# Top-32 attention and two MLPs: inverse row sums once per group, through HBM

## The chip, the cores and the metric

The kernel runs on one core of a Trainium2 chip. The metric is the device time of one execution in microseconds; three executions of the kernel before took 1342.15, 1345.45 and 1345.49 us, median 1345.45. Five engines take part: PE (TensorE: matmuls and transposes), DVE (VectorE), ACT (ScalarE), POOL (GpSimd) and SP (SyncE), which issues every DMA of this kernel. Each runs its own queue of instructions in the order written and waits for others by semaphores.

## The reference

```python
scores = scale * np.matmul(q, k.transpose(0, 1, 3, 2))        # (4, 8, 576, 576), head_dim 64
kth = np.partition(scores, -32, axis=-1)[..., -32:-31]
scores = np.where(scores >= kth, scores, -1e9)
scores = scores - np.max(scores, axis=-1, keepdims=True)
attn = np.exp(scores)
attn = attn / (np.sum(attn, axis=-1, keepdims=True) + 1e-09)
x = np.matmul(attn, v)            # heads side by side: (2304, 512)
y = (sigmoid(x @ w_gate) * (x @ w_val)) @ w_out               # d_ff 1536
out = np.maximum(y @ w_in, 0) ** 2 @ w_out2                   # d_ff 2048
```

All is float32. Only row sums of the exponentials concern us here: each query row of each head has one, and row q of x must be multiplied by its inverse.

## The kernel before

**Tiling.** The 2304 tokens are cut into five chunks of 320, 512, 512, 512 and 448 columns. x is kept with its 512 features on partitions (four head pairs, two heads of 64 features each) and tokens along the free dimension. A *group* (32 of them) is one head pair of one batch within a chunk, 2 to 7 blocks of 64 queries. A group is cut into *units* (80): 128 queries of both heads, or, where the number of blocks is odd, a last half unit of 64 queries. A full unit has two *tiles* (one per head, 128 queries on the partitions), a half unit one (64 queries of head 0 on partitions 0 to 63, of head 1 on 64 to 127). There are 144 tiles. `END[u]` is the last tile of unit u, `FINAL_UNIT[g]` the last unit of group g.

**Slots.** All engines run the same loop over 148 slots; slot s belongs to tile s, whose score matmul PE issues two slots ahead. DVE finds the 32 largest in slots s and s+1 (four MAX8, three MATCH_REPLACE). In slot s+2 ACT (`find_below`, `enlarge`), POOL (`mask`) and ACT (`exp`, which also gives the row sums, L528) make the exponentials. In slot END+3 PE transposes the unit (`turn`, nine transposes, L404), ACT copies the result to SBUF (`copy_pt`) and PE multiplies by v (`times_v`, L422 and L424).

**Normalisation before.** Exponentials put queries on partitions, x puts them along the free dimension, so the inverse must be turned as well. Per unit, in slot END+3: POOL adds 1e-9 (`add_eps`, L719), DVE inverts (`invert`, L649), POOL spreads the two inverses over 128 columns (`spread_inverse`, L729), PE transposes that (L412), in `times_v`, ahead of the products with v. It lands in the same PSUM bank, RR, as the product. In slot END+4 ACT copies both, 256 columns, to `rp` (`copy_pv`, L543), and POOL multiplies them into `xf` (`normalise`, L738; for a half unit two multiplies of 64x64, L743 and L746). When a pair has all its columns in a chunk, ACT and POOL split xf into a high and a low part (`split_x`, L555 and L752, at the slot in `X_AT`), the inputs of the three-pass products.

**MLP.** A chunk's products (68 weight blocks, each in two halves of six matmuls, L465 to L467) run beside the attention of the next chunk. `shares()` deals the 136 halves to the slots so that PE's work per slot is even by a cost formula written in the program; a slot's share has three parts (before the scores, before times_v, after it). Products of chunk c begin in slot `MLP_AT[c]` (23, 56, 88, 120, 147); the last chunk's, `REST`, run after the last slot. A block's results are evacuated by ACT, DVE and POOL, for the third part in the next slot. Weights are split into high and low parts once: for chunks 0 and 1 some blocks are split on the way (ACT L549, POOL L707) and stored to HBM (L322); otherwise both parts are loaded (L329) into a ring of four places, each when the block four before is done.

**Order on the engines around the change.** POOL in a slot: add_eps, normalise, mask, split_x, evac of the last third part, spread_inverse, split_head, split_weights, evac. ACT: copy_scores, find_below, copy_pv, enlarge, evac of the last third part, copy_pt, split_x, exp, split_head, split_weights, evac. SP: ring loads and stores of the last third part, loads of heads and v, raw weights and their stores, ring loads of parts one and two.

## Time and profile before

| | us |
|---|---|
| median of three executions | 1345.45 |
| profiled execution, its own time | 1344.6 |
| its span, first to last instruction | 1342.8 |
| DVE busy | 846.0 (63%) |
| ACT busy | 808.0 (60%) |
| POOL busy | 731.5 (54%) |

TensorE's mean granted clock was 0.94 of full speed. An engine's busy share says how full it is on average, and averages hide stages: the first stretch holds attention alone, the last one matmuls alone. Times "from 380 us" and the like count from the start of the span. A row of a group view reads: line, engine, operation, what it writes and reads, shape, count, then busy us and mean ns of one, then the idle time of the engine just ahead of them with what ended most of it.

### The profile page before, as it was taken

The page shows a single profiled execution, that of the slowest core. Times are in us where ns is not written, and L with a number is a line of the kernel's source. Part 1 is how long each engine was busy: PE and PEld are TensorE (multiplying, and loading weights), DVE is VectorE, ACT ScalarE, POOL GpSimd, SP SyncE. Part 2 cuts the span into 40 slices and gives each one's busy share as a digit, 9 for nine tenths or more (in the row PEclk, how much of TensorE's full clock was granted, in tenths as well). Part 3 has the DMA queues.
Part 4 walks back from the last instruction along what each step waited for, and adds up shares of the span by engine and source line. Part 5 has one row for each costly group of instructions (what it writes and reads, how often), then busy time and mean ns, then how long its engine had stood idle before and what let it go on. Part 6 is the DMA issues. An engine that isn't in the chain of part 4 may idle for free.

```text
span 1342.8 us, 20893 instructions
## 1 busy us (share of the span) xinstructions
PE 1205.0 (90%) x6960; PEld 1033.2 (77%) x6960; DVE 846.0 (63%) x1680; ACT 808.0 (60%) x1712; POOL 731.5 (54%) x785
## 2 busy tenths in 40 slices
PE   3465588887789999999999999999999999999999
PEld 3344487877687888877888888788888887889998
DVE  6767877777876775787757868875666676011130
ACT  5667777667776676777656657755565574311130
POOL 5766577777775664787536527854453553122130
PEclk9655789898899999999999999999999999999999
DMA  4666145555465556545655555656454544566665
GB/s 135 224 234 216 58 159 208 178 176 177 159 221 211 210 186 214 194 171 197 214 181 178 183 165 194 211 165 219 149 195 160 184 139 151 160 219 216 216 216 184
DMA packets 78873, 249.34 MB, mean 186 GB/s; under 512 B 8752, under 2 KB 9776, under 8 KB 78768
## 3 DMA queue, kind: packets, MB, share of 16 engines
q1 hardware_dynamic: 78768, 248.02, 54.3%
q8 instruction: 56, 0.92, 0.3%
q14 instruction: 49, 0.40, 0.1%
HBM read 207.62 MB, written 40.37 MB: 185 GB/s over the span
## 4 chain that ended last, share of the span: by engine, by line
PE 69%; POOL 16%; ACT 7%; issue 6%; DMA 2%; SPq 0%; POOLq 0%; ACTq 0%
PE ps L465 18%; PE ps L467 18%; PE ps L466 17%; PE ps L422 5%; PE ps L404 4%; PE ps L392 4%; POOL ring L707 4%; POOL below L712 4%; POOL klo L694 3%; POOL qkh L699 2%; PE ps L424 2%; ACT qkh L500 2%; POOL full_buf L773 1%; DMA w_raw<-w_in 1%; ACT scores L505 1%
## 5 line engine op out<-in xcount | busy, mean ns | idle before, releaser
L465 PE MATMUL ps<-xy_hi,ring 128*128 128x512 f32 (+2 forms) x800 | 306.1, 383 | 15.2 <-POOL ring L707 7.3
L633 DVE MAX8 top<-work 128x8 f32<-128x576 f32 x432 | 312.4, 751 | 5.0
L466 PE MATMUL ps<-xy_lo,ring 128*128 128x512 f32 (+2 forms) x800 | 297.5, 372 | 0.0
L467 PE MATMUL ps<-xy_hi,ring 128*128 128x512 f32 (+2 forms) x800 | 297.5, 372 | 0.0
L712 POOL TENSOR_TENSOR below<-scores,below 128x576 f32<-128x576 f32 x144 | 206.9, 1437 | 58.3 <-ACT below L517 51.1
L465 PE MATMUL ps<-g_hi,ring 128*128 128x512 f32 (+2 forms) x560 | 214.2, 382 | 7.7 <-POOL ring L707 7.5
L635 DVE MATCH_REPLACE8 work<-top,work 128x576 f32<-128x576 f32 x288 | 214.0, 743 | 0.0
L467 PE MATMUL ps<-g_hi,ring 128*128 128x512 f32 (+2 forms) x560 | 208.8, 373 | 0.0
L466 PE MATMUL ps<-g_lo,ring 128*128 128x512 f32 (+2 forms) x560 | 208.6, 373 | 0.0
L465 PEld LDWEIGHTS ps<-xy_hi,ring 128*128 128x128 f32 x800 | 152.6, 191 | 35.8 <-issue 8.6
L467 PEld LDWEIGHTS ps<-xy_hi,ring 128*128 128x128 f32 x800 | 151.8, 190 | 22.4
L466 PEld LDWEIGHTS ps<-xy_lo,ring 128*128 128x128 f32 x800 | 152.5, 191 | 17.3
L528 ACT ACTIVATE probs<-below,nbias 128x576 f32<-128x576 f32 x128 | 100.3, 784 | 103.0 <-POOL below L712 102.7
L694 POOL TENSOR_TENSOR klo<-raw,qkh 128x576 fp32r<-128x576 f32 x64 | 91.4, 1428 | 110.0 <-ACT qkh L500 109.8
L659 DVE SCALAR_TENSOR_TENSOR full_buf<-act_buf,ps 128x512 f32<-128x512 f32 (+2 forms) x60 | 37.9, 632 | 169.9 <-PE ps L467 163.2
L707 POOL TENSOR_TENSOR ring<-w_raw,ring 128x512 fp32r<-128x512 f32 x90 | 116.6, 1300 | 38.0 <-ACT ring L549 36.0
L763 POOL TENSOR_TENSOR g_lo<-full_buf,g_hi 128x512 fp32r<-128x512 f32 (+2 forms) x60 | 70.9, 1182 | 106.4 <-ACT g_hi L583 105.8
L670 DVE TENSOR_TENSOR g_lo<-full_buf,g_hi 128x512 fp32r<-128x512 f32 (+2 forms) x80 | 75.1, 939 | 82.6 <-ACT g_hi L587 82.6
L392 PE MATMUL ps<-qkh 128*128 128x288 f32 x320 | 101.2, 330 | 28.1 <-ACT scores L505 17.4
L773 POOL TENSOR_TENSOR full_buf<-act_buf 128x512 f32<-128x512 f32 (+2 forms) x80 | 83.2, 1042 | 76.4 <-ACT act_buf L576 74.4
L465 PEld LDWEIGHTS ps<-g_hi,ring 128*128 128x128 f32 x560 | 107.0, 191 | 21.6 <-POOL ring L707 4.6
L467 PEld LDWEIGHTS ps<-g_hi,ring 128*128 128x128 f32 x560 | 106.5, 190 | 15.8
(56 smaller groups left out, 2118.8 us busy)
## 6 DMA issues: line engine op xcount, KB each, us to landing
ring<-w_split SPq DMA_DIRECT2D x273, 512.0 KB, 3.4
w_split<-ring SPq DMA_DIRECT2D x68, 512.0 KB, 2.9
w_raw<-w_in SPq DMA_DIRECT2D x90, 256.0 KB, 3.5
vt<-v_in SPq DMA_DIRECT2D x32, 320.0 KB, 4.8
raw<-qk_in SPq DMA_DIRECT2D x16, 512.0 KB, 4.9
raw<-qk_in SPq DMA_DIRECT2D x16, 416.0 KB, 4.5
raw<-qk_in SPq DMA_DIRECT2D x8, 576.0 KB, 4.5
raw<-qk_in SPq DMA_DIRECT2D x8, 480.0 KB, 4.7
```

Of the source, the lines that this page charges most:

```text
L392: mm = nc.tensor.matmul(dst, qkh[:, r, at:at + P], rhs, start=(done == 0), stop=(done == steps - 1))
L465: nc.tensor.matmul(dst, w_hi, hi[:, k, 0:WIDTH[c]], start=(k == 0), stop=False)
L466: nc.tensor.matmul(dst, w_hi, lo[:, k, 0:WIDTH[c]], start=False, stop=False)
L467: mm = nc.tensor.matmul(dst, w_lo, hi[:, k, 0:WIDTH[c]], start=False, stop=(k == parts * KT - 1))
L528: last = nc.scalar.activation(probs_of(u)[rows, h, :], below[rows, t % 2, :], ACT.Exp, bias=nbias[rows, t % 4:t % 4 + 1], scale=SCALE, acc ...
L633: nc.vector.max(out=best, in_=sc if step == 0 else wk).then_inc(sel_step[t % 2], 1)
L635: nc.vector.match_replace(out=wk, in_to_replace=best, in_values=sc if step == 1 else wk, imm_value=-3.0e38).then_inc(sel_step[t % 2], 1)
L670: nc.vector.tensor_tensor(out=g_lo[:, j, 0:n_w], in0=full_buf[:, j % 2, 0:n_w], in1=g_hi[:, j, 0:n_w].bitcast(F32), op=ALU.subtract).then_ ...
L694: nc.gpsimd.tensor_tensor(out=klo[:, j % 4, :], in0=raw[:, j % 2, q:q + SEQ], in1=qkh[:, j % 4, q:q + SEQ].bitcast(F32), op=ALU.subtract). ...
L707: nc.gpsimd.tensor_tensor(out=place(k)[:, 1, :], in0=w_raw[:, r % RAW, :], in1=place(k)[:, 0, :].bitcast(F32), op=ALU.subtract).then_inc(w ...
L712: nc.gpsimd.tensor_tensor(out=below[:, t % 2, :], in0=scores[:, t % 4, :], in1=below[:, t % 2, :], op=ALU.subtract).then_inc(mask_done, 1)
L773: nc.gpsimd.tensor_tensor(out=full_buf[:, j % 2, 0:n_w], in0=act_buf[:, j % 2, 0:n_w], in1=act_buf[:, j % 2, 0:n_w], op=ALU.mult).then_inc ...
```

## The change

Per unit, PE no longer transposes inverses, and `copy_pv` copies 128 columns of the unnormalised product from PSUM straight into xf (for a half unit, two copies of 64x64). The row sums of a group are collected in 2 to 7 columns of `rsum`. Once per group: POOL adds 1e-9 and DVE inverts, at the end of its slot END+3 of the group's last unit; SP stores the inverses in slot END+4 to a table `inv` in HBM (queries along the row), and at the end of the same slot loads them back with two or four DMAs, each repeated over the 64 partitions of its head, into `rr`; POOL multiplies the group's columns of xf by `rr` in place, in slot END+5 (for group 3, the last of chunk 0, in slot END+4, which is slot 23).

The order of the engines' work moves too. POOL masks first, and evacuates before it normalises. ACT's copy_pv comes after enlarge and after evac of the last third part. X_AT follows the groups' normalisation: chunk 0's pairs are split in slots 9, 14, 19 and 23 (before: 8, 13, 18, 23), the last pairs of chunks 1, 2 and 3 in slots 56, 88 and 120 (before: 55, 87, 119). The last chunk's products start a slot later, so that the number of slots is 149. In slot 23 the whole share of products is put after times_v.

```diff
@@ -115,8 +125,8 @@
 
 
 
-MASK, TURN, NORM = 2, 3, 4
-MLP_AT = [CHUNK_END[c] + (4 if c in (0, NC - 1) else 5) for c in range(NC)]
+MASK, TURN, COPY = 2, 3, 4
+MLP_AT = [CHUNK_END[c] + (4 if c == 0 else 5) for c in range(NC)]
 SLOTS = MLP_AT[NC - 1] + 1
...
@@ -141,8 +151,7 @@
             upto = min(max(upto, done), 2 * NB)
             todo = [(c, h) for h in range(done, upto)]
             done = upto
-            a = (len(todo) + 1) // 3
-            b = (len(todo) + 1) // 3
+            a = b = 0 if s == MLP_AT[0] else (len(todo) + 1) // 3
             out[s] = (todo[:a], todo[a:a + b], todo[a + b:])
...
-HEADS_AT, X_AT = {}, {}
+HEADS_AT, NORM_AT, X_AT = {}, {}, {}
 for _g in range(1, NG):
     for _h in range(2):
         HEADS_AT.setdefault(max(FIRST_TILE[_g] - 4 + _h, 0), []).append((_g, _h))
+for _g in range(NG):
+    NORM_AT.setdefault(END[FINAL_UNIT[_g]] + (4 if _g == PAIRS - 1 else 5), []).append(_g)
 for _c in range(NC):
     for _p in range(PAIRS):
-        _s = END[X_UNIT[_c][_p]] + NORM
+        _s = next(s for s in NORM_AT if X_GROUP[_c][_p] in NORM_AT[s])
         X_AT.setdefault(_s if _c == 0 else max(_s, slot_of_block(_c - 1, OUT0 - 1) + 1), []).append((_c, _p))
...
+INV_AT = {END[FINAL_UNIT[g]]: g for g in range(NG)}
...
-        rsum = sb("rsum", [P, 2, 2])
-        rsum_eps = sb("rsum_eps", [P, 2, 2])
-        rinv = sb("rinv", [P, 2, 2])
-        rinv_q = sb("rinv_q", [P, 2, 2, B64])
+        rsum = sb("rsum", [P, 2, NBLK])
+        rsum_eps = sb("rsum_eps", [P, 2, NBLK])
+        rinv = sb("rinv", [P, 2, NBLK])
+        rr = sb("rr", [P, 2, NMAX])
         pt = sb("pt", [P, 2, NBLK * P])
-        rp = sb("rp", [P, 2, 2 * P])
...
+            def store_inverses(g):
+                n = sums_of(g)
+                sp.wait_ge(inv_done, g + 1)
+                sp.dma_start(inv[g, 0:n, :].rearrange("m q -> q m"), rinv[:, g % 2, 0:n],
+                             allow_slow_non_contiguous=True).then_inc(inv_stored, 16)
+
+            def load_inverses(g):
+
+                n = GROUPS[g][4] // 2
+                sp.wait_ge(inv_stored, 16 * (g + 1))
+                wait(sp, x_done, g - 1)
+                for h in range(2):
+                    rows = slice(DH * h, DH * h + DH)
+                    if n:
+                        sp.dma_start(rr[rows, g % 2, 0:P * n].rearrange("p (i q) -> p i q", q=P),
+                                     inv[g, h:2 * n:2, :].unsqueeze(0).to_broadcast([DH, n, P])).then_inc(
+                                         inv_loaded[g % 2], 16)
+                    if GROUPS[g][4] % 2:
+                        sp.dma_start(rr[rows, g % 2, P * n:P * n + B64],
+                                     inv[g, 2 * n:2 * n + 1, B64 * h:B64 * h + B64].to_broadcast([DH, B64])).then_inc(
+                                         inv_loaded[g % 2], 16)
...
             for s in range(SLOTS):
                 if s > 0:
                     mlp_dma(blocks_of(SHARES[s - 1][2]))
+                if s - COPY in INV_AT:
+                    store_inverses(INV_AT[s - COPY])
...
                 mlp_dma(blocks_of(SHARES[s][0] + SHARES[s][1]))
+                if s - COPY in INV_AT:
+                    load_inverses(INV_AT[s - COPY])
...
                 for k in range(NBLK):
-                    dst = ps[:, T0 + k // 4, P * (k % 4):P * (k % 4) + P] if k < 8 else ps[:, RR, 0:P]
-                    mm = nc.tensor.transpose(dst, both[:, P * k:P * k + P], ident[:, :])
+                    mm = nc.tensor.transpose(ps[:, T0 + k // 4, P * (k % 4):P * (k % 4) + P], both[:, P * k:P * k + P], ident[:, :])
                 mm.then_inc(transposed, 1)
 
             def times_v(u):
                 g = UNITS[u][1]
                 pe.wait_ge(pt_copied, u + 1)
-
-                pe.wait_ge(inv_spread, u + 1)
-                nc.tensor.transpose(ps[:, RR, 0:P], rinv_q[:, u % 2, :, :].rearrange("p h c -> p (h c)"),
-                                    ident[:, :]).then_inc(inv_turned, 1)
...
                 wait(act, transposed, u - 1)
-                wait(act, sum_done, u - 1)
+                wait(act, sum_done, g - 1)
...
                     rows = slice(B64 * h, B64 * h + B64) if part == 2 else slice(0, P)
-                    col = 0 if part == 2 else h
+                    col = 2 * i if part == 2 else 2 * i + h
                     last = nc.scalar.activation(probs_of(u)[rows, h, :], below[rows, t % 2, :], ACT.Exp,
                                                 bias=nbias[rows, t % 4:t % 4 + 1], scale=SCALE,
-                                                accum_out=rsum[rows, u % 2, col:col + 1])
...
             def copy_pv(u):
+                c, g, p, i, half, col = UNITS[u]
                 act.wait_ge(pv_done, u + 1)
-                wait(act, x_done, u - 1)
-                nc.scalar.activation(rp[:, u % 2, :], ps[:, RR, 0:PV + P], ACT.Copy).then_inc(pv_copied, 1)
+                if c > 0:
+
+                    act.wait_ge(x_lo_done, (c - 1) * NM + p + 1)
+                for h in range(2) if half else [2]:
+                    rows = slice(DH * h, DH * h + DH) if half else slice(0, P)
+                    at, n = (PV + B64 * h, B64) if half else (PV, P)
+                    last = nc.scalar.activation(xf[rows, p, col:col + n], ps[rows, TAIL, at:at + n], ACT.Copy)
+                last.then_inc(pv_copied, 1)
...
@@ -597,12 +638,12 @@
                     copy_scores(s + 1)
                 if 0 <= s - MASK < NT:
                     find_below(s - MASK)
-                if s - NORM in UNIT_AT:
-                    copy_pv(UNIT_AT[s - NORM])
                 if 0 <= s - MASK < NT:
                     enlarge(s - MASK)
                 for c, n in blocks_of(SHARES[s - 1][2]) if s else []:
                     evac(c, n)
+                if s - COPY in UNIT_AT:
+                    copy_pv(UNIT_AT[s - COPY])
                 if s - TURN in UNIT_AT:
                     copy_pt(UNIT_AT[s - TURN])
...
-            def invert(u):
-                heads = 1 if UNITS[u][4] else 2
-                dve.wait_ge(sum_done, u + 1)
-                wait(dve, inv_spread, u - 1)
-                nc.vector.reciprocal(rinv[:, u % 2, 0:heads], rsum_eps[:, u % 2, 0:heads]).then_inc(inv_done, 1)
+            def invert(g):
+                n = sums_of(g)
+                dve.wait_ge(sum_done, g + 1)
+                if g >= 2:
+                    dve.wait_ge(inv_stored, 16 * (g - 1))
+                nc.vector.reciprocal(rinv[:, g % 2, 0:n], rsum_eps[:, g % 2, 0:n]).then_inc(inv_done, 1)
...
@@ -676,12 +718,12 @@
                 select_both(s, [0, 1])
                 for c, n in blocks_of(SHARES[s - 1][2]) if s else []:
                     evac(c, n)
-                if s - TURN in UNIT_AT:
-                    invert(UNIT_AT[s - TURN])
                 select_both(s, [2])
                 for c, n in blocks_of(SHARES[s][0] + SHARES[s][1]):
                     evac(c, n)
                 select_both(s, [3])
+                if s - TURN in INV_AT:
+                    invert(INV_AT[s - TURN])
...
-            def add_eps(u):
-                heads = 1 if UNITS[u][4] else 2
-                pool.wait_ge(exp_done, END[u] + 1)
-                wait(pool, inv_done, u - 1)
-                nc.gpsimd.tensor_scalar(rsum_eps[:, u % 2, 0:heads], rsum[:, u % 2, 0:heads], 1e-9, None,
+            def add_eps(g):
+                n = sums_of(g)
+                pool.wait_ge(exp_done, END[FINAL_UNIT[g]] + 1)
+                wait(pool, inv_done, g - 1)
+                nc.gpsimd.tensor_scalar(rsum_eps[:, g % 2, 0:n], rsum[:, g % 2, 0:n], 1e-9, None,
                                         ALU.add).then_inc(sum_done, 1)
 
-            def spread_inverse(u):
-                pool.wait_ge(inv_done, u + 1)
-                wait(pool, inv_turned, u - 1)
-                if UNITS[u][4]:
-                    src = rinv[:, u % 2, 0:1].unsqueeze(2).to_broadcast([P, 2, B64])
-                else:
-                    src = rinv[:, u % 2, :].unsqueeze(2).to_broadcast([P, 2, B64])
-                nc.gpsimd.tensor_copy(rinv_q[:, u % 2, :, :], src).then_inc(inv_spread, 1)
-
-            def normalise(u):
-                c, g, p, i, half, col = UNITS[u]
-                pool.wait_ge(pv_copied, u + 1)
...
-                    pool.wait_ge(x_lo_done, (c - 1) * NM + p + 1)
-                if not half:
-                    nc.gpsimd.tensor_tensor(out=xf[:, p, col:col + P], in0=rp[:, u % 2, PV:PV + P],
-                                            in1=rp[:, u % 2, 0:P], op=ALU.mult).then_inc(x_done, 1)
...
-
-                pool.wait_ge(inv_spread, u + 1)
-                nc.gpsimd.tensor_tensor(out=xf[0:B64, p, col:col + B64], in0=rp[0:B64, u % 2, PV:PV + B64],
-                                        in1=rp[0:B64, u % 2, 0:B64], op=ALU.mult).then_inc(x_half_done, 1)
-                pool.wait_ge(x_half_done, RANK[u] + 1)
-                nc.gpsimd.tensor_tensor(out=xf[B64:P, p, col:col + B64], in0=rp[B64:P, u % 2, PV + B64:PV + P],
-                                        in1=rp[B64:P, u % 2, B64:P], op=ALU.mult).then_inc(x_done, 1)
-                pool.wait_ge(x_done, u + 1)
+            def normalise(g):
+                c, b, p, at, n, col = GROUPS[g]
+                pool.wait_ge(pv_copied, FINAL_UNIT[g] + 1)
+                pool.wait_ge(inv_loaded[g % 2], 16 * inv_loads(g))
+                x = xf[:, p, col:col + B64 * n]
+                nc.gpsimd.tensor_tensor(out=x, in0=x, in1=rr[:, g % 2, 0:B64 * n], op=ALU.mult).then_inc(x_done, 1)
...
             for s in range(SLOTS):
-                if s - TURN in UNIT_AT:
-                    add_eps(UNIT_AT[s - TURN])
-                if s - NORM in UNIT_AT:
-                    normalise(UNIT_AT[s - NORM])
                 if 0 <= s - MASK < NT:
                     mask(s - MASK)
+                if s - TURN in INV_AT:
+                    add_eps(INV_AT[s - TURN])
+                for c, n in blocks_of(SHARES[s - 1][2]) if s else []:
+                    evac(c, n)
+                for g in NORM_AT.get(s, []):
+                    normalise(g)
                 for c, p in X_AT.get(s, []):
                     split_x(c, p)
-                for c, n in blocks_of(SHARES[s - 1][2]) if s else []:
-                    evac(c, n)
-                if s - TURN in UNIT_AT:
-                    spread_inverse(UNIT_AT[s - TURN])
                 for g, h in HEADS_AT.get(s, []):
                     split_head(g, h)
...
```

## Rows read from the trace of the kernel before

**Rows 1.** The page, part 1: busy us (share of the span) xinstructions by engine.

```profile
PE 1205.0 (90%) x6960; PEld 1033.2 (77%) x6960; DVE 846.0 (63%) x1680; ACT 808.0 (60%) x1712; POOL 731.5 (54%) x785
```

**Rows 2.** Windows: length, busy PE, PEld, DVE, ACT, POOL, then PEclk, DMA share, GB/s.

```profile
0.00:170.00 170.00, 90.79 (x475) 73.68 (x476) 119.38 (x246) 113.68 (x237) 107.81 (x123) 0.68 0.50 171
170.00:380.00 210.00, 170.84 (x1195) 159.81 (x1194) 163.87 (x330) 151.76 (x340) 158.38 (x167) 0.91 0.52 181
380.00:1190.00 810.00, 793.55 (x4556) 661.22 (x4555) 539.08 (x1076) 512.30 (x1079) 438.82 (x470) 0.99 0.54 186
1190.00:1343.00 153.00, 149.82 (x740) 138.52 (x738) 23.62 (x29) 30.28 (x59) 26.46 (x26) 1.00 0.64 209
```

**Rows 3.** The chain of waits from 0 to 200 us, by line.

```profile
by line: issue 15.2%; POOL below L712 11.9%; POOL ring L707 11.9%; DMA w_raw<-w_in 7.9%; POOL klo L694 7.1%; POOL qkh L699 6.0%; ACT qkh L500 5.7%; PE ps L404 3.8%; ACT scores L505 3.0%; ACT below L510 2.7%; DMA raw<-qk_in 1.9%; PE ps L392 
```

**Rows 4.** PE's waits from 170 to 380 us: us in total, times, longest us.

```profile
PE ps L412 <- POOL rinv_q L729: 23.3, 9, 5.7
PE ps L465 <- POOL ring L707: 12.2, 6, 4.8
```

**Rows 5.** PE's waits from 380 to 1190 us.

```profile
PE ps L412 <- POOL rinv_q L729: 9.8, 5, 2.8
PE ps L465 <- DMA ring<-w_split: 1.1, 1, 1.1
```

**Rows 6.** Timeline of PE, two places: start us, us, engine, line, operation.

```profile
769.24 1.14 PE L404 MATMUL ps<-ident,probs 128*128 128x128 f32 x9
770.13 0.48 PE L465 MATMUL ps<-g_hi,ring 128*128 128x512 f32 x1
...
773.31 0.39 PE L467 MATMUL ps<-g_hi,ring 128*128 128x512 f32 x1
773.54 0.27 PE L412 MATMUL ps<-ident,rinv_q 128*128 128x128 f32 x1
773.74 1.09 PE L422 MATMUL ps<-pt,vt 128*64 128x128 f32 x16
```

**Rows 7.** Groups of POOL instructions, 170 to 380 us: busy us, mean ns, idle before.

```profile
L738 POOL TENSOR_TENSOR xf<-rp 128x128 f32<-128x128 f32 x14 | 6.7, 480 | 13.3 <-ACT rp L543 13.2
L729 POOL COPY rinv_q<-rinv 128x128 f32<-128x128 f32 x14 | 4.3, 309 | 0.1
L719 POOL TENSOR_SCALAR rsum_eps<-rsum 128x2 f32<-128x2 f32 x14 | 3.0, 213 | 1.2
```

**Rows 8.** Groups by form over the whole span.

```profile
L712 POOL TENSOR_TENSOR below<-scores,below 128x576 f32<-128x576 f32 x144 | 206.9, 1437 | 58.3 <-ACT below L517 51.1
L752 POOL TENSOR_TENSOR xy_lo<-xf,xy_hi 128x512 fp32r<-128x512 f32 x12 | 15.7, 1313 | 0.9 <-ACT xy_hi L555 0.9
L569 ACT ACTIVATE act_buf<-ps 128x512 f32<-128x512 f32 x36 | 21.4, 593 | 39.6 <-PE ps L467 39.6
L743 POOL TENSOR_TENSOR xf<-rp 64x64 f32<-64x64 f32 x16 | 5.5, 343 | 21.0 <-ACT rp L543 20.9
L752 POOL TENSOR_TENSOR xy_lo<-xf,xy_hi 128x320 fp32r<-128x320 f32 x4 | 3.5, 862 | 0.0
```

**Rows 9.** Timeline around slot 23.

```profile
164.43 0.39 ACT L543 ACTIVATE rp<-ps 128x256 f32<-128x256 f32 x1 [0.64 <-PE ps L424]
...
167.95 0.41 PE L465 MATMUL ps<-xy_hi,ring 128*128 128x320 f32 x1 [2.25 <-POOL xy_lo L752]
```

**Rows 10.** The page, parts 3 and 6: DMA queue, and issues with us to landing.

```profile
q1 hardware_dynamic: 78768, 248.02, 54.3%
...
ring<-w_split SPq DMA_DIRECT2D x273, 512.0 KB, 3.4
w_split<-ring SPq DMA_DIRECT2D x68, 512.0 KB, 2.9
```

**Rows 11.** SP's waits over the span.

```profile
SPq L322 <- POOL ring L707: 395.3, 67, 17.9
```

**Rows 12.** Timeline of SP's issues near 614 us.

```profile
614.46 0.33 SPq L318 DMA_DIRECT2D w_raw<-w_in  x1
```

More of the change, by code:

```diff
@@ L56, with sums_of, inv_loads @@
 RANK = [sum(UNITS[v][4] == UNITS[u][4] for v in range(u)) for u in range(NU)]
-X_UNIT = [[max(u for u in range(NU) if UNITS[u][0] == c and UNITS[u][2] == p) for p in range(PAIRS)] for c in range(NC)]
+X_GROUP = [[max(g for g in range(NG) if GROUPS[g][0] == c and GROUPS[g][2] == p) for p in range(PAIRS)] for c in range(NC)]
 CHUNK_END = [max(END[u] for u in range(NU) if UNITS[u][0] == c) for c in range(NC)]
+def sums_of(g):
+    return 2 * (GROUPS[g][4] // 2) + GROUPS[g][4] % 2
+def inv_loads(g):
+    return sum(2 * ((GROUPS[h][4] > 1) + GROUPS[h][4] % 2) for h in range(g % 2, g + 1, 2))
 def full_columns(g):
@@ L178, with attention_mlps @@
     SPLIT_AT.setdefault(3 + _i // 2, []).append(_k)
-def attention_mlps(nc, qk, v, w, w_split, out):
+INV_AT = {END[FINAL_UNIT[g]]: g for g in range(NG)}
+def attention_mlps(nc, qk, v, w, w_split, inv, out):
     with ExitStack() as ctx:
@@ L217, in attention_mlps @@
         ps = ctx.enter_context(nc.psum_tensor("ps", [P, 8, 512], F32))
-        T0, RR, PV, ACC0 = 2, 4, P, 5
+        T0, TAIL, PV, ACC0 = 2, 4, P, 5
         def s_ps():
@@ L264, in attention_mlps @@
         inv_done = sem("inv_done")
-        inv_spread = sem("inv_spread")
-        inv_turned = sem("inv_turned")
+        inv_stored = sem("inv_stored")
+        inv_loaded = [sem("inv_loaded0"), sem("inv_loaded1")]
         transposed = sem("transposed")
@@ L270, in attention_mlps @@
         pv_copied = sem("pv_copied")
-        x_half_done = sem("x_half_done")
         x_done = sem("x_done")
@@ L421, in times_v @@
                         p_at = P * ((KFULL + 1) * h + k)
-                        nc.tensor.matmul(ps[d, RR, PV:PV + P], vt[:, g % 2, v_at:v_at + DH],
+                        nc.tensor.matmul(ps[d, TAIL, PV:PV + P], vt[:, g % 2, v_at:v_at + DH],
                                          pt[:, u % 2, p_at:p_at + P], start=(k == 0), stop=False)
-                mm = nc.tensor.matmul(ps[:, RR, PV:PV + P], vt[:, g % 2, KFULL * DH:KFULL * DH + P],
+                mm = nc.tensor.matmul(ps[:, TAIL, PV:PV + P], vt[:, g % 2, KFULL * DH:KFULL * DH + P],
                                       pt[:, u % 2, P * KFULL:P * KFULL + P], start=False, stop=True)
@@ L537, in copy_pt @@
                 nc.scalar.activation(pt[:, u % 2, 512:1024], ps[:, T0 + 1, :], ACT.Copy)
-                nc.scalar.activation(pt[:, u % 2, 1024:NBLK * P], ps[:, RR, 0:P], ACT.Copy).then_inc(pt_copied, 1)
+                nc.scalar.activation(pt[:, u % 2, 1024:NBLK * P], ps[:, TAIL, 0:P], ACT.Copy).then_inc(pt_copied, 1)
             def copy_pv(u):
+                c, g, p, i, half, col = UNITS[u]
                 act.wait_ge(pv_done, u + 1)
-                wait(act, x_done, u - 1)
-                nc.scalar.activation(rp[:, u % 2, :], ps[:, RR, 0:PV + P], ACT.Copy).then_inc(pv_copied, 1)
+                if c > 0:
[5 more added lines that the diff above has]
+                last.then_inc(pv_copied, 1)
             def split_weights(k):
@@ L551, in split_x @@
             def split_x(c, p):
-                act.wait_ge(x_done, X_UNIT[c][p] + 1)
+                act.wait_ge(x_done, X_GROUP[c][p] + 1)
                 if c > 0:
@@ L589, in _ @@
             act.wait_ge(const_ready, 1)
-            nc.scalar.activation(rp[:, 0, 0:1], ident[:, 0:1], ACT.Exp)
+            nc.scalar.activation(rsum[:, 0, 0:1], ident[:, 0:1], ACT.Exp)
             split_head(0, 0)
@@ L847 @@
     w_split = nc.dram_tensor("w_split", (NB, P, 2 * KT * P), F32, kind="Internal").ap()
-    attention_mlps(nc, *aps, w_split, out)
+    inv = nc.dram_tensor("inv", (NG, NBLK, P), F32, kind="Internal").ap()
+    attention_mlps(nc, *aps, w_split, inv, out)
     r = run_bass_kernel_spmd(nc, [arrays], core_ids=[0])
```

4 lines of the change are left out of this document (2 added, 2 removed).

## The prediction, made before the result was known

> **What bounds the kernel now.** I read the page's busy times first: PE is busy 1205.0 of 1342.8 us [rows 1]. Then busy time by stretch [rows 2]: there are two regimes. From 380 us to the end of attention (1190) PE is busy 793.6 of 810 us, and after that only matmuls remain; there, what PE issues is what the kernel takes. Before 380 no engine is full. From 0 to 170 us (attention alone, slots 0 to 22) PE has 90.8, DVE 119.4, ACT 113.7, POOL 107.8; from 170 to 380 (chunk 0's products beside chunk 1's attention) PE has 170.8 of 210, DVE 163.9, POOL 158.4. The chain of waits for the first 200 us [rows 3] is led by POOL's mask and weight splits, by "issue" (hand-offs), and by DMA. So POOL's queue, in its order, sets the early pace. PE's own waits say the same: from 170 to 380 it stood 23.3 us at L412, the transpose of the spread inverse, for POOL's rinv_q, and 12.2 us for a weight split [rows 4]; after 380 only 9.8 us at L412 [rows 5].
>
> **The change, part by part.**
>
> *PE, after 380 us.* L412 goes, once per unit; 26 of its 80 executions start before 380 us (14 from 170 on, [rows 7], 12 before that), 54 after. In the gapless stream its start and the next matmul's are 773.54 and 773.74, so one is worth 0.20 us [rows 6]: 54 x 0.20 = 10.8 us off. The stalls in front of it (9.8 us) go too, but the matmuls behind may find a later cause; from 0 to 9.8 I take 6. Together -16.8.
>
> *POOL, 170 to 380.* Fourteen units lose add_eps (3.0 us), spread (4.3) and normalise (6.7), and normalise's 13.3 us of waiting for ACT's copy [rows 7]: 27.3. Seven groups of 256 columns gain an add_eps (0.21) and one normalise. No multiply of 128x256 is in the trace; it lies between 0.48 (128 columns, [rows 7]) and 0.86 (a subtraction of 320, [rows 8]); I take 0.74, near the upper. That is 6.7. POOL's queue gets 20.6 us shorter, but DVE's 163.9 and PE's 170.8 of 210 are close behind and ACT's hand-offs stay. Bounds 0 and 20.6; I take -12.
>
> *POOL, 0 to 170.* Twelve units, four of them half units with two 64x64 multiplies (0.34 each, [rows 8]): 12 x 0.52 + 8 x 0.48 + 4 x 0.68 = 12.8 off; on: 4 x (0.21 + 0.86) = 4.3. Net 8.5, of which the weight loads and ACT's chain hide part: bounds 0 and 8.5, taken -6. Here the mask also comes ahead of anything that waits for PE's product.
>
> *DVE and ACT.* The reciprocals fall from 80 to 32. DVE is no bound (846 of 1342.8 us busy), so I count nothing. ACT's copy shrinks from 256 to 128 columns (0.39 us before, [rows 9]), hidden beside PE after 380 and inside the halves taken above before it.
>
> *The round trip, where it is in the open.* Group 3 ends in slot 19, its inverse is ready at the end of DVE's slot 22, and slot 23 holds store, loads, normalise, split_x and the first matmul. Before, the copy was released at 164.4 and PE began chunk 0 at 167.95, after normalise, high and low split [rows 9]. Now a store must land before the loads are issued. No DMA so small is in the trace; big ones land in 2.9 us (store) and 3.4 (ring load) [rows 10]. Store and load are then 6.3, less the mask that runs beside (1.4, [rows 8]): +5, bounds 0 and 9. It stands in POOL's and ACT's queues: behind it are the splits of the next heads and exp of tile 21, and PE waits for both. In a sentence of its own: the Trainium skill ("DMA: Bandwidth & Descriptors", section "Anatomy of one DMA") gives every DMA about 2 us, mostly the receipt of the write, so by it the round trip would be 4 us and this term 2.6; the two landings in [rows 10] include moving 512 KB, so trace and rule do not contradict each other.
>
> *Other loads in POOL's way.* SP issues load_inverses at the end of its slot, after store_parts, and store_parts waits for POOL's weight split (395 us of SP waiting, [rows 11]). So in slots 8 and 13 and in chunk 0's product slots the loads start only when POOL ends that slot; POOL's next one holds a mask (1.4) and perhaps one block before normalise, against two issues of 0.33 us each [rows 12] and some 3.4 of landing. I take 2 us at slots 9 and 14 and 0.5 for each of eight groups: +8, bounds 0 and 20.
>
> *A new order on ACT.* copy_pv moves behind enlarge and behind the evacuation of the last slot's third share. In slots where a half unit follows at once, PE's turn waits for that very copy at the slot's start (its products share bank TAIL). After 380 there are 12 such slots; in 9 the third share ends in a block on which ACT has no work or in no block. In the other 3 (gate 8, h 14, h 8) ACT must evacuate (0.59, [rows 8]), make a high part of like length and copy (about 0.3), with hand-offs 1.7 us: +5, bounds 0 and 12.
>
> *Starts of chunks 1 to 3.* normalise and split_x of the last pair now stand in the very slot (56, 88, 120) in which PE starts the chunk. PE gets to the second half block, which needs the pair, after nine transposes (769.24 to 770.13), six matmuls of 0.23 [rows 6] and a score: 2.8 us. ACT takes the transposes' copies (about 1.5 us) first, then the high split (near the evacuation's 0.59), then POOL 1.31 [rows 8]: 0.9 + 1.5 + 0.6 + 1.3 + 0.2 = 4.5. Stall 1.7 each, 5 in all. The last chunk's start moves a slot back: loads after the second share, 4 + 1.1 + 0.6 + 1.1 = 6.8 us (multiply, high split and low split of 448 columns, from the rows of 320 and 512), against 4.1 of third share and 1.8 of matmuls that don't need this pair: +1. Bounds 0 and 12 together.
>
> *SP and the DMA queues.* The store writes sums that lie 4 bytes in a partition to addresses 512 bytes apart: 128 x (2 to 7) pieces, none next to another. Over 32 groups that is 18,432 pieces, and the loads are 10,240 of 256 or 512 bytes, on top of 78,768. Price of a 4-byte packet: the trace has none alone; below it costs nothing, above it costs as much as the mean one, 54.3% x 16 x 1342.8 / 78,768 = 0.148 us [rows 10]. A store with 5 sums is 40 packets in each of 16 queues: 0 to 5.9 us ahead of a ring load. A ring load has three blocks to land, 3 x 12 x 0.23 = 8.3 us, less its 3.4: 4.9 in hand. I take a third of the upper price, so 2 us (2.8 for 7 sums): hidden after 380, +2 in all before it. Again by itself: the Trainium skill (same page, "Specifications") says transfers under 512 bytes are a read-modify-write and lose line rate; no row here shows one. If that brought the price to the upper bound, it is the second rival below.
>
> **The sum**: -16.8 - 12 - 6 + 5 + 8 + 5 + 6 + 2 = -8.8. The profiled execution took 1344.6 us (span 1342.8 and 1.8 around it), 0.85 under the median 1345.45. So 1336.6; I say 1336.
>
> **Rivals.**
> 1. *POOL was the whole early bound.* Then its relief counts fully (-20.6 - 8.5), all L412 stalls go (-9.8), and the loads arrive in time (+2 in place of 8, +4 in place of 11): -10.8 - 9.8 - 29.1 + 5 + 2 + 4 + 2 = -37, about 1308. For: 23.3 us of PE waits for POOL at one line. Against: DVE at 164 of 210.
> 2. *The store's packets delay the ring loads (slower).* At 0.148 us the stores of groups 12 to 15 (5.9 us), 20 to 23 (7.1) and 28 to 31 (8.3) exceed the 4.9 in hand by 1.0, 2.2 and 3.4 us, four times each: 26, and some 8 for raw weight loads before 380. 1336 + 34 = 1370. It decides from 4.9 / 56 = 0.09 us per packet. For: a DMA share of 0.54 after 380 [rows 2] with queues shared by all loads. Against: the payload is nearly nothing.
> 3. *POOL's relief is worth nothing* (ACT's chain and DVE hold the early pace) and the round trips stay: -16.8 + 26 = +9, 1355. For: 'issue' and DMA in [rows 3]. Against: [rows 4].
> 4. *Gains and costs cancel*: half of the relief taken, everything added as summed: 1345.
>
> **Chances.** Forecast 0.45, rival 1 0.17, rival 4 0.17, rival 2 0.10, rival 3 0.11. What a measurement can tell from no change is 0.3%, or 4 us. Faster by more than that 0.62, within 0.17, slower 0.21. The range 1314 to 1357 leaves out most of rivals 1 and 2.
>
> **What would show it.** PE from 380 on: no L412, stream gapless before L422, and its length about 11 us less; stalls at L404 for ACT's copy in three slots, at L465 for xy_lo in slots 56, 88, 120. In slot 23 PE's start of chunk 0 relative to the last product's end: 3.5 us before, some 8.5 after. POOL's normalise waiting for DMA in slots 9 and 14. The attention-only stretch shorter by a few us, 170 to 380 by 5 to 12. The landing time of the store (over 5 us speaks for rival 2) and PE's waits for ring loads (1.1 us after 380, [rows 5]) would overturn it, as would an early stretch of unchanged length.

## The result: 1506 us, 12% slower, and the profile after

The changed kernel takes 1506.11 us (median of four executions, 1500.35 to 1507.95), the kernel before 1345.24: a ratio of 1.119, 95% interval 1.116 to 1.123. The prediction said 1336 and 1357 at most.

Windows of the changed kernel, to be read beside [rows 2] (length, busy PE, PEld, DVE, ACT, POOL, PEclk, DMA share, GB/s; its span is 1504.6 us):

```profile
0.00:170.00 170.00, 75.96 (x378) 62.20 (x378) 107.92 (x217) 97.77 (x204) 90.17 (x80) 0.63 0.60 170
170.00:380.00 210.00, 143.89 (x969) 133.86 (x969) 125.54 (x258) 125.13 (x281) 116.82 (x108) 0.83 0.58 134
380.00:1190.00 810.00, 709.01 (x4013) 588.35 (x4014) 514.40 (x1002) 480.16 (x1030) 398.61 (x338) 0.94 0.63 172
1190.00:1505.00 315.00, 300.35 (x1521) 260.79 (x1519) 94.33 (x159) 102.11 (x215) 78.73 (x69) 0.98 0.62 182
```

Before, PE was busy 90.8, 170.8 and 793.6 us in the first three windows; now 76.0, 143.9 and 709.0. No engine took over the work: PE, DVE, ACT and POOL are all less busy in each of the three. Only the DMA share rose (0.54 to 0.63 after 380 us) while the GB/s fell (186 to 172). PE's waits over the span (us in total, times, longest):

```profile
PE ps L430 <- ACT scores L538: 63.4, 20, 10.8
PE ps L498 <- DMA ring<-w_split: 49.0, 19, 9.6
PE ps L498 <- POOL xy_lo L773: 34.8, 5, 14.0
PE ps L441 <- ACT xf L583: 33.1, 13, 5.1
```

They have no single cause: PE stands for scores, for ring loads, for x's low part and for the copied product. Gone, as forecast, is its longest wait of the kernel before:

```profile
PE ps L412 <- POOL rinv_q L729: 49.1, 24, 5.7
```

Now who holds the other engines. POOL's wait ahead of normalise, and SP's ahead of the loads:

```profile
POOL xf L769 <- DMA rr<-inv: 259.2, 31, 27.8
```

```profile
SPq L373 <- DMA inv<-rinv: 141.7, 28, 8.6
```

POOL stood 259 us for the returned inverses, in 31 of 32 groups, and SP 142 us for the stores to land. The chain of work that ended last, by line (the page's part 4), says it too:

```profile
DMA inv<-rinv 14%; PE ps L498 11%; PE ps L499 11%; PE ps L500 11%; DMA rr<-inv 7%; DMA ring<-w_split 6%; POOL ring L749 3%; POOL klo L736 3%; PE ps L441 3%; POOL below L754 3%; POOL qkh L741 2%; PE ps L430 2%; PE ps L455 2%; ACT qkh L533 2%; DMA w_raw<-w_in 1%
```

Here "DMA inv<-rinv" is the store. One round trip in the timeline, group 3 in slot 23 (start us, us, engine, line, operation), against [rows 9]:

```profile
182.26 0.19 DVE L691 RECIPROCAL rinv<-rsum_eps 128x5 f32<-128x5 f32 x1 [5.64 <-POOL rsum_eps L761]
182.47 0.38 SPq L362 DMA_DIRECT2D inv<-rinv  x1
182.89 0.52 SPq L319 DMA_DIRECT2D raw<-qk_in  x1
...
193.91 0.61 SPq L373 DMA_DIRECT2D rr<-inv  x1
...
198.96 0.86 POOL L769 TENSOR_TENSOR xf<-xf,rr 128x320 f32<-128x320 f32 x1 [10.97 <-DMA rr<-inv]
199.85 0.47 ACT L596 ACTIVATE xy_hi<-xf 128x320 fp32r<-128x320 f32 x1 [13.03 <-POOL xf L769]
200.40 0.86 POOL L773 TENSOR_TENSOR xy_lo<-xf,xy_hi 128x320 fp32r<-128x320 f32 x1 [0.58 <-ACT xy_hi L596]
201.31 0.64 PE L498 MATMUL ps<-xy_hi,ring 128*128 128x320 f32 x1 [13.99 <-POOL xy_lo L773]
```

The store is issued at 182.47 and SP can issue the first load at 193.91, 11.4 us later; the inverses are in at 199. PE, through nine of the twelve matmuls of its first block, stood 14.0 us where it stood 2.25 before. POOL stood 11.0 us and ACT 13.0, and behind them are the masks and exponentials of the tiles in work. In all 32 groups the first load is issued 8.8 to 12.8 us after the store. SP has other work in between, so this bounds the landing from above, but 28 times the store is what SP stood for last.

The stall has a second price. The same 320-column matmul before and behind it:

```profile
186.00 0.31 PE L499 MATMUL ps<-xy_lo,ring 128*128 128x320 f32 x1
...
201.75 0.47 PE L499 MATMUL ps<-xy_lo,ring 128*128 128x320 f32 x1
```

From 201.3 to 205 us the granted clock is 0.57 of full speed, near the lower of its two levels (1.2 and 2.4 GHz); from 205 to 210 it is 1.00 again. What that adds up to is counted below, at no_round_trip. DMA of the page, against [rows 10]:

```profile
q1 hardware_dynamic: 109488, 252.82, 61.4%
...
ring<-w_split SPq DMA_DIRECT2D x273, 512.0 KB, 3.8
...
vt<-v_in SPq DMA_DIRECT2D x32, 320.0 KB, 11.0
```

The v loads, which SP issues right behind a store, land in 11.0 us in the median (4.8 before).

### The profile page after: what moved, and what is told of

Same layout as the page of the kernel before. It is cut to its first block, busy times and chain, and to the rows that moved or that the text cites. A ratio compares the mean times of both kernels' runs of the same rounds, so it can differ in the third digit from the quotient of the medians.

```text
span 1504.6 us, 20395 instructions
## 1 busy us (share of the span) xinstructions
PE 1229.2 (82%) x6880; PEld 1045.2 (69%) x6880; DVE 842.2 (56%) x1632; ACT 805.2 (54%) x1728; POOL 684.3 (45%) x593
## 4 chain that ended last, share of the span: by engine, by line
PE 40%; DMA 28%; POOL 13%; ACT 8%; SPq 5%; issue 5%; DVE 0%; ACTq 0%; POOLq 0%
DMA inv<-rinv 14%; PE ps L498 11%; PE ps L499 11%; PE ps L500 11%; DMA rr<-inv 7%; DMA ring<-w_split 6%; POOL ring L749 3%; POOL klo L736 3%; PE ps L441 3%; POOL below L754 3%; POOL qkh L741 2%; PE ps L430 2%; PE ps L455 2%; ACT qkh L533 2%; DMA w_raw<-w_in 1%
## 5 line engine op out<-in xcount | busy, mean ns | idle before, releaser
L498 PE MATMUL ps<-xy_hi,ring 128*128 128x512 f32 (+2 forms) x800 | 313.9, 392 | 99.9 <-DMA ring<-w_split 35.7
L499 PE MATMUL ps<-xy_lo,ring 128*128 128x512 f32 (+2 forms) x800 | 303.9, 380 | 0.0
L500 PE MATMUL ps<-xy_hi,ring 128*128 128x512 f32 (+2 forms) x800 | 303.1, 379 | 0.0
L498 PEld LDWEIGHTS ps<-xy_hi,ring 128*128 128x128 f32 x800 | 156.6, 196 | 127.1 <-issue 56.0
L498 PE MATMUL ps<-g_hi,ring 128*128 128x512 f32 (+2 forms) x560 | 217.3, 388 | 25.9 <-DMA ring<-w_split 13.3
L500 PE MATMUL ps<-g_hi,ring 128*128 128x512 f32 (+2 forms) x560 | 210.9, 377 | 0.0
L500 PEld LDWEIGHTS ps<-xy_hi,ring 128*128 128x128 f32 x800 | 156.3, 195 | 23.2
L499 PEld LDWEIGHTS ps<-xy_lo,ring 128*128 128x128 f32 x800 | 157.1, 196 | 17.9
L430 PE MATMUL ps<-qkh 128*128 128x288 f32 x320 | 105.5, 342 | 73.3 <-ACT scores L538 63.4
L769 POOL TENSOR_TENSOR xf<-xf,rr 128x320 f32<-128x320 f32 (+5 forms) x32 | 25.6, 801 | 259.3 <-DMA rr<-inv 259.2
L674 DVE MAX8 top<-scores 128x8 f32<-128x576 f32 x144 | 107.3, 745 | 61.6 <-ACT scores L538 61.6
L498 PEld LDWEIGHTS ps<-g_hi,ring 128*128 128x128 f32 x560 | 109.4, 195 | 42.1 <-issue 14.4
L712 DVE TENSOR_TENSOR g_lo<-full_buf,g_hi 128x512 fp32r<-128x512 f32 (+2 forms) x80 | 75.8, 948 | 109.7 <-ACT g_hi L628 109.6
L430 PEld LDWEIGHTS ps<-qkh 128*128 128x128 f32 x320 | 70.3, 220 | 83.6 <-issue 72.6
```

The source lines that it names most:

```text
L430: mm = nc.tensor.matmul(dst, qkh[:, r, at:at + P], rhs, start=(done == 0), stop=(done == steps - 1))
L498: nc.tensor.matmul(dst, w_hi, hi[:, k, 0:WIDTH[c]], start=(k == 0), stop=False)
L499: nc.tensor.matmul(dst, w_hi, lo[:, k, 0:WIDTH[c]], start=False, stop=False)
L500: mm = nc.tensor.matmul(dst, w_lo, hi[:, k, 0:WIDTH[c]], start=False, stop=(k == parts * KT - 1))
L674: nc.vector.max(out=best, in_=sc if step == 0 else wk).then_inc(sel_step[t % 2], 1)
L712: nc.vector.tensor_tensor(out=g_lo[:, j, 0:n_w], in0=full_buf[:, j % 2, 0:n_w], in1=g_hi[:, j, 0:n_w].bitcast(F32), op=ALU.subtract).then_ ...
```

## Experiments

The theories about the time lost: **A**, the round trip comes late into queues that work in order; **B**, the store's 4-byte packets hold up all other transfers; **C**, the new order on ACT and POOL and the later starts of the chunks cost the time; **D**, the loads are late by themselves. Each run's time is a median; the kernel before took 1345.0 to 1345.6 beside them.

**no_round_trip**: the whole change but its DMAs and the waits on them; x is multiplied by a constant, so the result is not the reference's.

```diff
-                    store_inverses(INV_AT[s - COPY])
-                    load_inverses(INV_AT[s - COPY])
-                pool.wait_ge(inv_loaded[g % 2], 16 * inv_loads(g))
+            nc.gpsimd.memset(rr[:, :, :], 1.0)
```

> The changed kernel without the store, the loads and the waits on them; x is multiplied by a constant tile instead of the inverses. What is left is the gain side and the new order of work. Theory A (the round trip of the inverses is late, and POOL and SP stand in order behind it) and theory B (the store's 4-byte packets hold up all other transfers) both expect the sum of my prediction without its DMA terms: 1320 us, from 1305 to 1335. Theory C (the new order on POOL and ACT and the later starts of the chunks cost the time) expects over 1450.

Measured: 1324.5 us, ratio 0.985 (0.983 to 0.988): 20.5 us faster than before, where A and B expected it. C falls. Its windows, and PE's waits between 380 and 1175 us:

```profile
0.00:170.00 170.00, 89.55 (x459) 74.02 (x460) 122.27 (x246) 114.28 (x242) 101.38 (x91) 0.73 0.50 171
170.00:380.00 210.00, 179.28 (x1246) 168.61 (x1246) 167.19 (x333) 157.25 (x354) 156.38 (x142) 0.91 0.55 191
380.00:1190.00 810.00, 792.05 (x4526) 658.93 (x4525) 530.73 (x1028) 506.58 (x1084) 406.53 (x339) 1.00 0.54 188
```

```profile
PE ps L437 <- ACT xf L579: 9.9, 8, 2.3
PE ps L494 <- POOL xy_lo L766: 1.3, 2, 0.7
PE ps L494 <- DMA ring<-w_split: 0.2, 1, 0.2
```

From 170 to 380 PE does 8.4 us more work than before in the same stretch, and of the stalls I had charged, little more than the one for ACT's copy is there (9.9 us). Over the whole span, though, other waits of PE have grown:

```profile
PE ps L426 <- ACT scores L534: 30.9, 18, 3.2
PE ps L437 <- ACT xf L579: 23.0, 12, 3.9
PE ps L451 <- ACT pt L568: 15.7, 16, 2.2
```

In the kernel before, the waits for these three were 17.4, 6.2 and 0.4 us. So 45.6 us came back of the 49.1 that went with L412.

This run also tells how the 182 us between it and the changed kernel divide, as PE has the same instructions in both. Part 1 of the page (busy us, share of the span, instructions), in the changed kernel and then here:

```profile
PE 1229.2 (82%) x6880; PEld 1045.2 (69%) x6880; DVE 842.2 (56%) x1632; ACT 805.2 (54%) x1728; POOL 684.3 (45%) x593
```

```profile
PE 1193.5 (90%) x6880; PEld 1024.1 (77%) x6880; DVE 842.0 (64%) x1632; ACT 804.4 (61%) x1728; POOL 687.3 (52%) x594
```

Of the 179 us between the two profiled spans PE stood 143 longer, and for 36 it was busy longer with the same work, at a mean granted clock of 0.90 against 0.95.

**store_only**: the stores without the loads.

```diff
 (against no_round_trip)
+                    store_inverses(INV_AT[s - COPY])
+                    dve.wait_ge(inv_stored[g % 2], 16 * (g // 2))
```

> As no_round_trip, but the 32 stores of the inverses are issued where they were; nobody waits for them but DVE, two groups later. No loads; x is multiplied by a constant tile. Theory A: within 10 us of no_round_trip. Theory B: most of the 185 us between 1320 and 1506 comes back, over 1430.

Measured: 1393.8 us. Neither expectation: 69 us over no_round_trip, so B is real and less than half of the 182 us to explain. The DMA queue and the v loads, first in no_round_trip, then here:

```profile
q1 hardware_dynamic: 78768, 248.02, 53.7%
...
vt<-v_in SPq DMA_DIRECT2D x32, 320.0 KB, 4.7
```

```profile
q1 hardware_dynamic: 97712, 248.10, 62.8%
...
vt<-v_in SPq DMA_DIRECT2D x32, 320.0 KB, 11.1
```

18,944 packets more (18,432 pieces, and 16 for each of the 32 stores) took (62.8% x 1389.7 - 53.7% x 1325.6) x 16 = 2,570 us of the engines, 0.136 us each for 4 bytes. The same sum differs by some 200 us between the kernel before and order_only (below; 54.3% and 53.4%), whose DMAs are the same, so the price is good to about 0.01 us.

**store_only_act_queue**: store_only with the same stores issued by ACT, behind copy_pt.

```diff
 (against store_only)
-                sp.dma_start(inv[g, 0:n, :].rearrange("m q -> q m"), ...
+                act.dma_start(inv[g, 0:n, :].rearrange("m q -> q m"), ...
```

> store_only (1394, v loads landing in 11.1 us against 4.7 without the store), with the same 4-byte stores issued from ACT's DMA queue instead of SP's, at the same slot after copy_pt. If the transfers behind a store are late because they stand behind it in the same queue, they pass it now: v loads near 5 us and 1325 to 1345. If the packets occupy the 16 DMA engines whichever queue they come from: the loads stay late and the time over 1375.

Measured: 1421.6 us. Another queue doesn't help, it costs 28 us more. PE was busy 21.5 us longer than in store_only (1218.6 against 1197.1), at a mean granted clock of 0.92 against 0.94; what brought that about no run settles. The two queues:

```profile
q1 hardware_dynamic: 78768, 248.02, 61.7%
q10 hardware_dynamic: 18944, 0.08, 0.8%
```

This is the clearest row on B. The 18,944 small packets of q10 are recorded with 0.8% of the time, 10 ns each; but q1's 78,768 packets, the same as in no_round_trip, take 61.7% x 1422.5 in place of 53.7% x 1325.6: 2,650 us of the engines more. So the price of the small writes is recorded in the others' packets.

**loads_only**: the loads without the stores, reading w in place of inv. What comes back are not the inverses.

```diff
-                sp.wait_ge(inv_stored, 16 * (g + 1))
-                                     inv[g, h:2 * n:2, :].unsqueeze(0)...
+                                     w[g, h:2 * n:2, 0:P].unsqueeze(0)...
```

> The changed kernel without the stores; the same 96 loads in the same places, waited for by POOL as before, but reading the weights' tensor, so that SP waits for no store. The values in rr are not the inverses. Theory A, with the store's 11 us in the trace as the price: POOL's wait for the loads falls from 259 us to under 60, and the time to 1320 to 1350. Theory B: the same, since the packets of the store are gone. Theory D (the loads themselves, issued at the end of SP's slot, are the late part): over 1400.

Measured: 1360.4 us, 36 over no_round_trip; POOL still stood 87 us:

```profile
POOL xf L764 <- DMA rr<-w_in: 87.4, 27, 21.2
```

A expected POOL under 60 us and at most 1350, and D over 1400: all missed. So a part of D holds: issued at the end of SP's slot, with 3.3 us to land in the median, loads are late for a multiply in the next slot.

**store_rows**: 128 packets per store, of 8 to 28 bytes, to neighbouring addresses. The inverses land in the wrong columns.

```diff
-                sp.dma_start(inv[g, 0:n, :].rearrange("m q -> q m"), rinv[:, g % 2, 0:n],
+                sp.dma_start(inv[g, :, :].rearrange("m q -> (m q)")[0:P * n].rearrange("(q m) -> q m", q=P),
+                             rinv[:, g % 2, 0:n]).then_inc(inv_stored, 16)
```

> The changed kernel with the store's pieces joined: each partition writes its 2 to 7 sums as one piece of 8 to 28 bytes to neighbouring addresses, 128 packets in place of 256 to 896. The loads read the same bytes in their old pattern, so the values land in the wrong columns. If the store's 10 to 12 us are a price per packet, it lands in 3 to 5 us and the time falls below 1400. If they are a fixed price of a small store from 128 partitions (in the trace groups with 2 sums take as long as groups with 7), it stays within 20 us of 1506.

Measured: 1368.6 us, 137 under the changed kernel, for the same bytes, so the price is not a fixed one of a small store. The store lands in 4 us, with 5 sums and with 7:

```profile
inv<-rinv SPq DMA_DIRECT2D x8, 2.5 KB, 4.0
...
inv<-rinv SPq DMA_DIRECT2D x4, 3.5 KB, 4.0
```

This edit changes two things, the number of pieces and how far apart they land; no run parts them.

**store_sp_waits**: SP stands for the landing, POOL does not.

```diff
 (against store_only)
                 mlp_dma(blocks_of(SHARES[s][0] + SHARES[s][1]))
+                    sp.wait_ge(inv_stored, 16 * (INV_AT[s - COPY] + 1))
```

> As store_only (1394 us), and SP waits at the end of the store's slot until the store has landed, as in the changed kernel; no loads, and POOL waits for nothing. The difference to store_only is the price of SP's queue standing still before the next ring loads. If SP's place in line is the larger part of what is still missing to 1506: over 1440. If POOL's wait for late values is: under 1410.

Measured: 1396.3 us, 2.5 over store_only, within its noise. SP's standing cost nothing here, but it stood for the stores only 34.8 us,

```profile
SPq L341 <- DMA inv<-rinv: 34.8, 14, 5.4
```

against 141.7 in the changed kernel. So the run speaks for POOL's wait as the larger part of what lies between 1394 and 1506, and does not exclude that a longer standing of SP costs something. In the changed kernel PE's waits for ring loads, where that would show, are 49.0 us against 45.6 in store_only.

**The two cures, apart and together.** normalise_later: the changed kernel with `(5 if _g == PAIRS - 1 else 6)` in NORM_AT and `(5 if c == 0 else 6)` in MLP_AT. turned_store:

```diff
+                dve.wait_ge(recip_done, g + 1)
+                nc.vector.transpose(out=rinv_t[:, g % 2, :], in_=rinv[:, g % 2, :]).then_inc(inv_done, 1)
...
+                for k in range(4):
+                    sp.dma_start(inv[g, 0:n, 32 * k:32 * k + 32],
+                                 rinv_t[32 * k:32 * k + n, g % 2, :]).then_inc(inv_stored, 16)
```

turned_store_later has both.

> The changed kernel with its 4-byte store as it was; only POOL's multiply stands one slot later and the chunks' products start a slot later. Of the 182 us between no_round_trip (1324.5) and the changed kernel (1506), store_only showed 69 for the packets alone, which stay. If the rest is POOL waiting for late values, it goes: 1385 to 1410. If a slot of some 8 us doesn't cover store and loads together (11 + 4 us): 1430 to 1470. If the slot's position is not the matter: within 15 us of 1506.

> The changed kernel with the store turned on DVE first (4 DMAs of 2 to 7 packets of 128 bytes) and POOL's multiply in its early slot END+5. With 128 packets (store_rows) the time was 1368.6. If what is left there is the loads' lateness, it stays: 1355 to 1372, as loads_only with no store at all took 1360. If the 128 packets still cost: under 1350.

> The changed kernel, computing the same result, with two cures: DVE turns the inverses in 32x32 blocks, so that the store is 4 DMAs of 2 to 7 packets of 128 bytes; and POOL multiplies one slot later (END+6, chunk 0's last group in END+5), with the chunks' products starting a slot later. If the store's pieces and the loads' lateness were all of the 182 us above no_round_trip (1324.5), this is near it: 1325 to 1345, at or under the kernel before. If the extra DMAs' issue on SP and the later starts cost: 1350 to 1370, like store_rows (1369).

Measured, us:

| | multiply in END+5 | one slot later |
|---|---|---|
| 4-byte pieces | 1506.1 | 1438.0 |
| pieces of 128 bytes | 1363.7 | 1331.0 |

POOL's wait for the inverses in normalise_later, and PE's for ring loads there; then POOL's in turned_store_later:

```profile
POOL xf L769 <- DMA rr<-inv: 52.6, 11, 29.7
```

```profile
PE ps L498 <- DMA ring<-w_split: 68.5, 28, 10.4
```

```profile
POOL xf L774 <- DMA rr<-inv: 22.8, 2, 21.8
```

Each cure alone is worth 142 and 68 us, together 175. The later slot takes POOL's wait from 259 to 53 us and leaves what the packets do: PE waits 68 us for ring loads. It is also 44 us above store_only, more than the first expectation allowed: POOL's remaining 53 us and 165 us of SP standing for the stores are both candidates, and no run parts them. With both cures, 6.5 us of the 182 remain above no_round_trip, with all 96 loads and their issues in place, so these cost little when nobody waits for them. That kernel gives the reference's result, 1% faster than before (0.991, 0.989 to 0.992).

With the multiply in END+5 and the loads in place there are now four amounts of pieces in 32 stores:

| pieces | run | us |
|---|---|---|
| none | loads_only | 1360.4 |
| 576 of 128 bytes | turned_store | 1363.7 |
| 4,096 of 8 to 28 bytes | store_rows | 1368.6 |
| 18,432 of 4 bytes | the changed kernel | 1506.1 |

The price is not proportional: 4,096 pieces cost 8 us, 4.5 times as many cost 146. Up to a landing of 4 us the store adds little to the loads' own lateness.

**order_only and dve_spread**: what the gain was made of. order_only is the kernel before with `mask` first on POOL, `normalise` behind `evac`, and `copy_pv` behind `enlarge` and `evac`. dve_spread keeps the old order:

```diff
-                pe.wait_ge(inv_spread, u + 1)
+                pe.wait_ge(inv_done, u + 1)
-                nc.vector.reciprocal(rinv[:, u % 2, 0:heads], rsum_eps[:, u % 2, 0:heads])...
+                nc.vector.reciprocal(rinv_q[:, u % 2, :, :], src)...   # src: rsum_eps, each sum 64 times
-                    spread_inverse(UNIT_AT[s - TURN])
```

> The kernel before with the change's order of work alone: POOL masks first, evacuates ahead of normalise; ACT copies the product after enlarge and evac. Inverses per unit through PE as before. no_round_trip lies 20.5 us under the kernel before. If that gain came from the removed work (POOL's three instructions and PE's transpose per unit): 1340 to 1350 here, perhaps worse, as PE waits for ACT's copy in slots of half units. If it came from the order: under 1335.

> The kernel before in its own order, with the same result, but POOL's spread_inverse is gone: DVE's reciprocal reads the sum 64 times over and writes the 128 columns itself, and PE waits for DVE instead of POOL. PE stood 49 us at this transpose for POOL's copy, 33 of them between 170 and 1190 us. If those waits and POOL's queue are the early bound: 1325 to 1338. If PE only waits for something else then: 1340 to 1348.

Measured: 1344.7 (ratio 0.9996, 0.998 to 1.001) and 1333.2 (0.992, 0.991 to 0.993). PE's waits at L412 and for ACT's copy in order_only, then at L412 in dve_spread:

```profile
PE ps L412 <- POOL rinv_q L729: 47.7, 23, 4.0
PE ps L404 <- ACT rp L543: 14.5, 12, 2.9
```

```profile
PE ps L412 <- DVE rinv_q L651: 12.7, 8, 2.4
PE ps L412 <- ACT pt L538: 11.5, 12, 2.0
```

The order brings nothing measurable; taking POOL's copy from between PE and the inverse brings 12 us, and PE's wait at L412 drops from 49 to 24 us. That is more than half of the 20.5 us that the whole change had to give, with no DMA at all.

**turned_later_copy_first**: `copy_pv` straight behind `find_below` again.

> turned_store_later (1331.0) with ACT's copy of the product back at its old place, straight behind find_below. There PE waits 21 us in 9 slots of half units for that copy (6 us in 4 in the kernel before). If these waits are on the path: 1318 to 1327. If the copy in front delays enlarge and mask by as much: 1329 to 1335.

Measured: 1327.6 us (0.987, 0.985 to 0.989), half a us above the first expectation, 3.4 under turned_store_later, and the fastest version here that gives the reference's result. PE's wait for the copy, before this edit and with it:

```profile
PE ps L444 <- ACT xf L586: 21.1, 9, 4.1
```

```profile
PE ps L444 <- ACT xf L586: 12.7, 5, 3.5
```

## Why the prediction was wrong

The steps without DMA held as a sum: -16.8 - 12 - 6 + 5 + 6 = -23.8, and no_round_trip measured -20.5. Their terms fit less well. L412 and its stalls are gone, but most of those 49.1 us returned at other lines: PE stood 132.1 us in place of 137.8, and was busy 11.5 less. The copy's stall was 9.9 us between 380 and 1175 (5 forecast). At the starts of chunks 1 to 3 PE stood 1.3 for the low part (5 forecast); at a chunk's start it can do nine matmuls, not six, before it needs the last pair. POOL's relief, -18 in the sum, was not measured by itself. So part of the closeness is luck.

The step that failed is "SP and the DMA queues". I bounded a 4-byte packet by 0 and 0.148 us, took a third, and found it hidden in the 4.9 us that a ring load has in hand. Measured in store_only: 0.136, close to the end that I had left to rival 2, whose point of decision was 0.09. But rival 2, at 1370, was too small as well: it counted only ring loads delayed by more than their slack, after 380 us mostly, and came to 34 us. The packets alone cost 69.

The larger part is that the two DMA steps were priced apart. "The round trip" took 2.9 + 3.4 us from transfers that are 200 times bigger and have 128 packets, as though a small store had to be quick. It took 11.4 + 5 in slot 23, of which the four issues of the loads took 3.1 (I had charged two of 0.33 elsewhere and none here), and PE's stall grew by 11.7 us there, not 5. "Other loads in POOL's way" took 8 us in all; the loads alone cost 36. And a store that lands in 9 to 13 us makes the values late in 31 of 32 groups: from store_only (1394) to the changed kernel there are 112 us more, of which the loads' own 36 would be a third, if the parts add up. Nor had the sum a term for the clock: of what was lost, 36 us are the same matmuls taking longer. My packet count and packet price, multiplied (40 x 0.148 = 5.9 us, plus a landing), would have given a store of nearly 9 us: I held that number against the ring loads and never against the store's own landing.

One row was misread as well. In [rows 9], 167.95 is not where PE began chunk 0. Nine matmuls of its first block had started by then, this one first, and the tenth waited:

```profile
164.15 0.39 PE L465 MATMUL ps<-xy_hi,ring 128*128 128x320 f32 x1
```

Counted from the last product's end, as the sign was, the tenth came 3.5 us later before and 15.9 after, not 8.5. The sum is not touched by this.

The Trainium skill had a rule for this that I did not weigh ("VectorE: DVE Perf Modes", section "The three transpose paths"): a plain DMA copy that transposes by its access pattern is 19 times slower than the DMA's own transpose when the innermost stride of the destination is large. No run here uses the DMA's own transpose, so none shows the factor. What the runs show is that turning the inverses on DVE first, 0.21 us a group, saved 142 us. And the 2 us that the prediction quotes from the Trainium skill ("DMA: Bandwidth & Descriptors", section "Anatomy of one DMA") are fitted there for DMAs that GpSimd issues; SP issues these, and in the median the small loads landed in 3.3 us (loads_only), the stores of 128 pieces in 4.0 (store_rows).

```profile
L696 DVE STREAM_TRANSPOSE rinv_t<-rinv 128x32 f32<-128x32 f32 x32 | 6.8, 212 | 1.1
```

No view of the profile could have settled rival 2's premise, since no 4-byte packet was in it; my fault was the choice within the bounds, and the range, which should have reached what the upper bound gave to both the queues and the landing. Open: why a store with 2 sums (16 packets in each queue) seems to land no sooner than one with 7 in the changed kernel, where packets times price would have it land much sooner; how much of the 112 us is SP's standing; and what in the engines the small writes hold up.

## What to carry to other kernels

Count a DMA's pieces, not only its bytes, and charge them three times: to the transfers around it, to its own landing, and to whoever waits for it in order. Where the pieces come from a transpose, turn the data on an engine ahead of the store, as DVE did here in 32x32 blocks. Give a value that comes back through HBM slack behind both of its DMAs: one slot more was worth 33 us here even with the quick store (1363.7 to 1331.0). And ask first whether the wait to be removed can be shortened in place, as moving one small copy from POOL to DVE did here.

## What the runs showed of the hardware

Packets of 4 bytes written to HBM cost the 16 DMA engines 0.14 us each, from SP's queue and from ACT's alike (store_only, store_only_act_queue). On ACT's queue, where they can be told apart, they are themselves recorded with 10 ns, and the rest is in the others' packets. By the same working, against loads_only, it is 0.16 us in the changed kernel and 0.19 in normalise_later. And a reciprocal on DVE is dear per element: 0.16 us for 2 columns (the kernel before), 0.95 us for 128 (dve_spread),

```profile
L651 DVE RECIPROCAL rinv_q<-rsum_eps 128x128 f32<-128x128 f32 x80 | 75.8, 947 | 81.1 <-POOL rsum_eps L721 80.6
```

so that dve_spread gained 12 us although it gave DVE 63 us of work more (75.8 against 12.8); inverting first and spreading with a copy was not tried.
